# Moving four small tensors behind the ring of rounded ELU tiles in a gated scan and ELU feed-forward kernel

## The reference

```python
sig = 1.0 / (1.0 + np.exp(-f_logit))
f = lower_bound + (1.0 - lower_bound) * sig
h = f[:, t] * h + (1 - f[:, t]) * x[:, t]        # for every t
h = x @ w_in
g = np.where(h > 0.0, h, np.exp(np.minimum(h, 0.0)) - 1.0)
out = g @ w_out
```

## Time and profile before

| | |
|---|---|
| median of 3 runs | 1008.64 us (1008.42 to 1009.03) |
| the profiled execution, device time | 1008.46 us |
| its span, first to last instruction | 1006.6 us |
| TensorE matmuls busy | 1001.7 us, 4362 instructions |
| weight loads busy | 817.3 us |
| ScalarE, VectorE, GpSimd busy | 791.6, 731.0, 631.4 us |
| DMA traffic | 41.88 MB, mean 42 GB/s |

### The profile page before, as it was taken

The page is one execution under the profiler, slowest core; times in us unless marked ns, Lnnn a source line. Parts: engine busy times, 40 slices in busy tenths (PEclk is TensorE's granted clock), DMA queues, the critical chain, the costliest instruction groups (busy, mean ns, idle before and its releaser), DMA issues.

```text
span 1006.6 us, 15352 instructions
## 1 busy us (share of the span) xinstructions
PE 1001.7 (100%) x4362; PEld 817.3 (81%) x4362; DVE 731.0 (73%) x915; ACT 791.6 (79%) x1425; POOL 631.4 (63%) x474
## 2 busy tenths in 40 slices
PE   9999999999999999999999999999999999999998
PEld 6888888888888888888888888888888888888997
DVE  6995876886786697588679668758867957875544
ACT  7987878777877877877787787787778778778775
POOL 2586887567557557656755855765675575566454
PEclk9999999999999999999999999999999999999999
DMA  7112002101201100210210120011021011000001
GB/s 272 63 32 63 33 1 74 53 1 52 73 0 42 52 31 0 73 52 0 63 63 0 42 63 21 18 55 52 0 64 61 0 46 64 5 0 9 36 1 37
DMA packets 23211, 41.88 MB, mean 42 GB/s; under 512 B 2704, under 2 KB 4240, under 8 KB 23184
## 3 DMA queue, kind: packets, MB, share of 16 engines
q1 hardware_dynamic: 22752, 41.04, 12.6%
q10 hardware_dynamic: 432, 0.53, 0.2%
HBM read 29.10 MB, written 12.45 MB: 41 GB/s over the span
## 4 chain that ended last, share of the span: by engine, by line
PE 99%; DMA 1%; ACT 0%; SPq 0%; DVE 0%; issue 0%
PE acc L862 18%; PE acc L860 18%; PE acc L861 17%; PE h L834 14%; PE h L832 14%; PE h L836 14%; PE h L956 1%; PE h L957 1%; PE h L955 1%; DMA w_in_raw<-w_in 1%; PE h L927 0%; PE h L936 0%; PE acc L927 0%; PE acc L956 0%; PE acc L957 0%; PE acc L955 0%
## 5 line engine op out<-in xcount | busy, mean ns | idle before, releaser
L315 POOL TENSOR_TENSOR g_lo<-e,g_hi 128x512 fp32r<-128x512 f32 (+1 forms) x384 | 518.6, 1359 | 369.5 <-ACT g_hi L456 369.3
L442 ACT ACTIVATE e<-h 128x512 f32<-128x512 f32 (+1 forms) x380 | 225.6, 594 | 166.2 <-PE h L836 135.0
L692 DVE SCALAR_TENSOR_TENSOR e<-e,h 128x512 f32<-128x512 f32 (+1 forms) x380 | 257.1, 677 | 77.3 <-ACT e L448 77.1
L862 PE MATMUL acc<-g_hi,w_out_lo 128*128 128x512 f32 (+1 forms) x768 | 301.9, 393 | 0.0
L860 PE MATMUL acc<-g_hi,w_out_hi 128*128 128x512 f32 (+1 forms) x768 | 301.0, 392 | 0.0
L861 PE MATMUL acc<-g_lo,w_out_hi 128*128 128x512 f32 (+1 forms) x768 | 299.7, 390 | 0.0
L456 ACT CAST g_hi<-e 128x512 fp32r<-128x512 f32 (+1 forms) x384 | 232.2, 605 | 20.7 <-DVE e L692 20.7
L448 ACT ACTIVATE e<-e 128x512 f32<-128x512 f32 (+1 forms) x384 | 241.6, 629 | 8.4
L834 PE MATMUL h<-a_lo,w_in_hi 128*128 128x512 f32 (+1 forms) x616 | 240.8, 391 | 0.0
L832 PE MATMUL h<-a_hi,w_in_hi 128*128 128x512 f32 (+1 forms) x616 | 240.0, 390 | 0.0
L836 PE MATMUL h<-a_hi,w_in_lo 128*128 128x512 f32 (+1 forms) x616 | 238.7, 388 | 0.0
(11 more groups left out here) (72 smaller groups left out, 569.7 us busy)
## 6 DMA issues: line engine op xcount, KB each, us to landing
out<-out_sb SPq DMA_DIRECT2D x44, 256.0 KB, 2.0
gate<-forget_logit SPq DMA_DIRECT2D x43, 256.0 KB, 2.7
x<-value SPq DMA_DIRECT2D x43, 256.0 KB, 2.7
w_in_raw<-w_in SPq DMA_DIRECT2D x8, 256.0 KB, 6.5
w_out_raw<-w_out SPq DMA_DIRECT2D x8, 256.0 KB, 7.4
x<-value SPq DMA_DIRECT2D x4, 224.0 KB, 2.5
gate<-forget_logit SPq DMA_DIRECT2D x4, 224.0 KB, 2.5
out<-out_sb SPq DMA_DIRECT2D x4, 224.0 KB, 2.0
```

Of the source, the lines that this page charges most:

```text
L315: nc.gpsimd.tensor_tensor(g_lo[:, t % RING, 0:w], e[:, t % TILES, 0:w], g_hi[:, t % RING, 0:w].bitcast(F32), ALU.subtract).then_inc(g_lo_r ...
L442: nc.scalar.activation(e[:, i, 0:w], bank_of(j, t)[:, 0:w], ACT.Relu, scale=-1.0).then_inc(r_ready, 1)
L692: nc.vector.scalar_tensor_tensor(e[:, t % TILES, 0:w], e[:, t % TILES, 0:w], -1.0, bank_of(j, t)[:, 0:w], ALU.add, ALU.max).then_inc(g_rea ...
L862: done = nc.tensor.matmul(bank, lo, g_hi[:, t % RING, 0:w], start=False, stop=closes)
```

## The change

Four allocations are moved: `carry`, `bound`, `slope` and `offset` come behind `g_lo`, and `e`, `p5`, `g_hi` and `g_lo` follow directly on `a4_lo`. Sizes, types, instructions and their order stay as they are.

```diff
--- before.py
+++ after.py
@@ -103,15 +103,14 @@
             w_plain_low.append(nc.alloc_sbuf_tensor_at(f"w_plain_lo{p}", [P, 4, P], F32R, offset=at))
         a4_hi = sb("a4_hi", [P, TILE], F32R)
         a4_lo = sb("a4_lo", [P, TILE], F32R)
+        e = sb("e", [P, TILES, TILE])
+        p5 = sb("p5", [P, TILE])
+        g_hi = sb("g_hi", [P, RING, TILE], F32R)
+        g_lo = sb("g_lo", [P, RING, TILE], F32R)
         carry = sb("carry", [P, BATCH, HALVES, 1])
         bound = sb("bound", [P, HALVES])
         slope = sb("slope", [P, HALVES])
         offset = sb("offset", [P, HALVES])
-
-        e = sb("e", [P, TILES, TILE])
-        p5 = sb("p5", [P, TILE])
-        g_hi = sb("g_hi", [P, RING, TILE], F32R)
-        g_lo = sb("g_lo", [P, RING, TILE], F32R)
 
 
         h = ctx.enter_context(nc.psum_tensor("h", [P, 4, TILE], F32))
```

## The result

| | before | after |
|---|---|---|
| median | 1008.53 us (1008.38 to 1009.03, 4 runs) | 992.37 us (991.91 to 992.92, 4 runs) |
| profiled execution, device time and span | 1008.46, 1006.6 us | 992.92, 991.1 us |
| first second product starts at | 18.61 us | 19.65 us |
| block 0 from there to block 1 | 71.96 us | 71.57 us |
| blocks 1 to 10 | 832.42 us | 816.73 us |

The ratio is 0.9839, with a 95% interval of 0.9822 to 0.9856: 16.2 us less. The prediction was 991.8. The granted clock was 1.00 in every profiled execution. By stretches the span's 15.5 us are: the start +1.0 us, block 0 -0.4, the full blocks -15.7, block 11 -0.5.

What follows compares the result with a forecast made beforehand. TensorE was taken as the bound, by the distance between matmul starts. From the profiled 1008.46 us, -16.6 -1.3 +0.3 +0.8 gave 991.7, predicted as a median of 991.8 us, with an 8-in-10 range of 989.5 to 1001.

Steps and rivals of the forecast that it cites:

- The main step (1): Blocks 1 to 10: all 3600 matmuls at 226.6 ns, 815.8 us in place of 832.4, a gain of 16.6 us.
- Block 0 (2): Block 0 from the first g: 312 matmuls at 226.6 ns, 70.7 us in place of 71.96, a gain of 1.3 us.
- The last block (3): Last block, 448 columns: g products go from 204.2 to 206.7 ns; together a loss of 0.3 us.
- The other engines (4): e and p5 moved for the other engines: at most 37 ns per operation either way, hidden from TensorE, cost nothing.
- VectorE's stretch (5): VectorE's tightest stretch in each full block: P4 of pair 2 about 0.08 us late, ten times, a loss of 0.8 us.
- No change: Second products: position is not the cause of their slower steps, so 1008.6 us; chance 0.11.
- Worse at 128: Ring at 128: about 2112 second products lose 2.5 ns each, +5.3 us, 1013.9 us; chance 0.07.
- Half of it: Only part of the second products' gain comes, or VectorE's stretch costs 8.4 us: about 1000 us; chance 0.08.

Runs made afterwards that it cites:

- without the waits: Kernel after, with VectorE's opening of the gate for batch 1, half 0 moved from pair 2 to pair 3, behind the scan: 991.67 us in one run.
- the alternating groups: Stand-alone matmul kernel, weights and/or operands alternating between remainders 128 and 256, against both always at 128: 228.7 (steady 228.3) to 232.0 ns a step, against 226.7.
- With it restored: Kernel after with the gate opening moved to pair 3 and block 0's first weights' subtraction moved behind tile 26's ELU: 990.10 us, against 992.32 for the kernel after.
- The sweep: Stand-alone kernel, groups of 60 matmuls, only the operand's or weights' start bytes changed: 226.7 to 234.4 ns a step at 512 columns, 200.0 to 206.7 at 448.
- the halves of the change: Two kernels against the kernel after: only g_hi and g_lo at 128, 992.61 us; only e and p5 at 128, 1007.93 us in one run.

## Why the prediction was right, and where it was not

**The main step (1), right in size.** 3600 matmuls at 226.6 ns were to take 815.8 us and take 816.0 without the waits (ten blocks of 81.60). The reason given, a distance between operand and weights modulo 512, was right in kind, with 256 in place of 512. That it is the load of the next weights that clashes was put forward as unshown, and is so still: the alternating groups speak against the simple form of it. The forecast put the gain under the second products and took one run of first products behind them, 228.3 ns, as nearly undisturbed; over the full blocks they took 229.6, and 5.0 of the 16.4 us were theirs. The sum was safe from this because it was taken over all 3600 matmuls at once.

**Block 0 (2), wrong.** The gain was to be 1.3 us and was 0.4. The step assumed that TensorE never waits in block 0 once it goes faster. In the kernel before, the ELU of tile 26 was over at 77.76 us, 0.34 us before the matmul that needs its bank (the two lines of before above); taken from the first second product, VectorE is at the same point in both kernels (58.5 us), and TensorE would now be there 1.0 us sooner. I checked VectorE's margin in the full blocks and not here, where it is as small. With it restored, block 0 gains 1.24 us.

**The last block (3), wrong in sign.** A loss of 0.3 us was forecast, the gain was 0.5. The 206.7 ns of the earlier trace rows were taken as the price of the place, and the first products as unchanged. But the six matmuls read there were the slowest run of their kind: the block's first products took 204.3 ns on average before. After, they take 202.3 and the second ones 202.9, and of the 0.5 us gained 0.34 are of the first products, which had been put at nothing. The sweep shows that equal remainders can have 202.7 or 206.7 at 448 columns, by what ran before; whether the kernel before met this, or the slowing by neighbours at another place as in its full blocks, no run separates. The 30 matmuls of 512 columns gained 0.07 us in place of 0.2, since they now stand among those of 448 at 230 ns.

**The other engines (4), right.** e and p5 alone change nothing, and GpSimd's subtraction still takes 1380 ns (1378 before), so the 37 ns had nothing to do with the place.

**VectorE's stretch (5), right to the detail.** 0.08 us per block, from P4 of pair 2, ten times: measured 81.68 against 81.60 us in nine of the ten blocks, 0.7 us. It did not show in the waits under TensorE, as the forecast of what would be seen had it, but as idle time of the weight path (0.21 us, "<-DVE h L685").

**The sum.** Forecast -16.6 -1.3 +0.3 +0.8 = -16.8 against the profiled execution; measured in the same stretches -16.4 -0.4 -0.5 +0.7 = -16.6. The errors of steps 2 and 3, 0.9 and 0.8 us, cancelled, and that was luck. The profiled execution of the kernel after shows only 15.5 because of its start: TensorE waits there twice for rounded activations, 0.9 us in all, where it waited once, and the first second product starts at 19.65 us. The ten profiles of the kernels of this shape have 18.2 to 19.7 without a pattern that their edits explain.

**The rule of the Trainium skill** ("TensorE: Matmul & The Clock Gate", the step on LDWEIGHTS in Part 2), that the load of the next weights takes no read bandwidth from the running matmul, would have made the change worth nothing. The sweep differs from what would follow by it: with nothing but bytes of distance changed, the step goes from 226.7 to 233.3 ns. The measurement decides; whether the two reads meet in a port or elsewhere no run here shows.

**The rivals.** "No change" fell to the halves of the change and to the sweep. "Worse at 128" fell with it: at 512 columns no place is better than equal remainders. "Half of it" did not come; its part about VectorE did in small (0.7 us of 8.4), and neighbours at two different places do slow each other, before the change and with the ring at 192, but nothing of that is left once all places are equal.

## What to carry to other kernels

Where TensorE never waits, look at the distance between matmul starts, not at durations: two families of one shape with different steps may point to where their operands lie, and a sweep by itself can tell. Take averages over many runs of matmuls: one run of six misled step 3. For float32r matmuls with new 512-byte weights each time and 512 columns, give moving operands and weights the same remainder modulo 256 bytes, which costs nothing but the order of allocations; for other column counts measure, since the best place differs. And when the bound engine gains 1.6%, read again every margin of the engines behind it, in the start-up block too: two stretches with less than 0.4 us of margin gave back 1.6 us here, and moving two VectorE operations got them back.

## What had not been expected of the hardware

- At 512 columns the distance counts modulo 256 bytes: 226.7 ns at 0 and 256, 228.9 at 64, 232.4 to 234.4 at the other multiples of 32, 236.9 at 4 bytes.
- The best step found was the column count plus 32 cycles of 2.4 GHz at 512, 480, 448 and 384 columns (226.7, 213.3, 200.0, 173.3 ns), each at another set of distances; at 256 columns it was less, 117.8 ns, where this sum gives 120.0.
- At 448 columns and distance 0 the steady step is 202.7 or 206.7 ns, by what ran before the stream.
- Two families of places in one stream affect each other: with g 128 bytes off (before), the unmoved first products take 229.6 ns on average, with g 64 bytes off 231.6, and the kernel is at 1006.7 us; alone at their place they take 226.7.
